# The first GEMM's leaky step on ScalarE's parametric rectifier, and attention's scales as a column

## The reference

```python
scores = q @ k.T / 8                       # 24 heads, 448 x 448, head_dim 64
scores = cap * tanh(scores / cap)          # cap = 30
x = softmax(scores) @ v                    # 896 x 768
h = x @ w_in                               # 768 x 2048: the first GEMM
g = maximum(0.01 * h, h)                   # the leaky step
x = g @ w_out                              # 2048 x 768: the second GEMM
xn = x / rms(x) * rms_g
out = (silu(xn @ w_gate) * (xn @ w_val)) @ w_out2   # 768 x 1536 twice, then 1536 x 768
```

## Time and profile before

| | us |
|---|---|
| median of 3 runs | 585.69 |
| lowest, highest | 584.68, 587.48 |
| the profiled execution | 586.64 |
| its span | 584.8 |
| PE busy | 571.6 (98%) |
| DVE busy | 386.7 (66%) |
| ACT busy | 261.2 (45%) |
| POOL busy | 273.2 (47%) |

### The profile page before, as it was taken

How to read it: one execution, slowest core, us unless ns; L and a number is a source line. 1 busy time by engine, 2 the same in 40 slices (tenths; PEclk the granted TensorE clock), 3 DMA queues, 4 the chain that set the end, 5 groups by cost and what they waited for, 6 DMA issues and landing times.

```text
span 584.8 us, 7734 instructions
## 1 busy us (share of the span) xinstructions
PE 571.6 (98%) x2805; PEld 491.1 (84%) x2805; DVE 386.7 (66%) x516; ACT 261.2 (45%) x428; POOL 273.2 (47%) x236
## 2 busy tenths in 40 slices
PE   5999999999999999999999999999999999999997
PEld 3555455599899999999999988999999999999997
DVE  4269798489978767334975498988888888511120
ACT  5787787414333344334643455443444434311110
POOL 1016455287855553333853477756687865100000
PEclk9999999999999999999999999999999999999999
DMA  6253442121311131111211011412111114100001
GB/s 166 78 184 110 126 122 62 34 72 55 108 55 54 55 109 59 55 53 28 78 54 54 0 56 54 163 59 92 67 54 55 55 54 139 52 27 28 28 27 55
DMA packets 30005, 41.48 MB, mean 71 GB/s; under 512 B 17040, under 2 KB 18960, under 8 KB 29968
## 3 DMA queue, kind: packets, MB, share of 16 engines
q1 hardware_dynamic: 29824, 40.99, 22.1%
q10 hardware_dynamic: 144, 0.00, 0.0%
HBM read 38.15 MB, written 2.80 MB: 70 GB/s over the span
## 4 chain that ended last, share of the span: by engine, by line
PE 87%; DVE 8%; issue 3%; DMA 1%; ACT 1%; DVEq 0%
PE ps L1325 38%; PE ps L1372 19%; PE ps L1449 15%; PE ps L1276 8%; PE ps L1257 3%; PE ps L1280 2%; PE ps L1261 1%; DVE s_sum L902 1%; DMA capc<-in_cap 1%; DVE x_lo L1080 1%; DVE g L955 1%; DVE s_sum L896 1%; DMA sums<-x_raw 1%; DVE x_raw L835 0%; DVE x_lo L1058 0%
## 5 line engine op out<-in xcount | busy, mean ns | idle before, releaser
L495 POOL TENSOR_TENSOR w_lo<-w_raw,w_hi 128x384 fp32r<-128x384 f32 x92 | 107.8, 1175 | 139.0 <-ACT w_hi L608 138.7
L1325 PE MATMUL ps<-x_hi,w_hi 128*128 128x448 f32 x420 | 154.5, 368 | 1.9 <-DVE a_t L918 1.1
L1325 PE MATMUL ps<-x_hi,w_lo 128*128 128x448 f32 x420 | 153.8, 366 | 0.0
L1325 PE MATMUL ps<-x_lo,w_hi 128*128 128x448 f32 x420 | 153.8, 366 | 0.0
L495 POOL TENSOR_TENSOR w_lo<-s_sum,w_hi 128x384 fp32r<-128x384 f32 x80 | 90.1, 1133 | 50.5 <-ACT w_hi L608 50.3
L1325 PEld LDWEIGHTS ps<-x_hi,w_hi 128*128 128x128 f32 x420 | 78.9, 188 | 10.6 <-issue 2.4
L1325 PEld LDWEIGHTS ps<-x_hi,w_lo 128*128 128x128 f32 x420 | 78.9, 188 | 6.9
L1325 PEld LDWEIGHTS ps<-x_lo,w_hi 128*128 128x128 f32 x420 | 78.9, 188 | 6.7
L608 ACT ACTIVATE w_hi<-s_sum 128x384 fp32r<-128x384 f32 x80 | 41.5, 523 | 81.2 <-PE ps L1325 67.7
L1276 PE MATMUL ps<-probs,v_ones 128*128 128x448 f32 x144 | 57.2, 547 | 0.9 <-DVE x_raw L835 0.8
L608 ACT ACTIVATE w_hi<-w_raw 128x384 fp32r<-128x384 f32 x92 | 47.2, 515 | 13.5 <-PE ps L1325 13.0
(11 more groups left out here) (141 smaller groups left out, 923.6 us busy)
## 6 DMA issues: line engine op xcount, KB each, us to landing
w_raw<-in_w_out SPq DMA_DIRECT2D x24, 384.0 KB, 3.1
w_raw<-in_w_in SPq DMA_DIRECT2D x16, 384.0 KB, 3.7
qk_raw<-in_qk SPq DMA_DIRECT2D x11, 480.0 KB, 4.2
w_raw<-in_w_gate SPq DMA_DIRECT2D x12, 384.0 KB, 3.0
w_raw<-in_w_val SPq DMA_DIRECT2D x12, 384.0 KB, 3.6
v_ones<-in_v SPq DMA_DIRECT2D x12, 224.0 KB, 3.2
recip_row<-recips SPq DMA_DIRECT2D x12, 224.0 KB, 3.3
v_raw<-in_w_out SPq DMA_DIRECT2D x4, 384.0 KB, 5.8
```

The source lines that it names most:

```text
L495: pool.tensor_tensor(w_lo[:, c], source, w_hi[:, c].bitcast(F32), ALU.subtract).then_inc(w_lo_done, 1)
L1325: last = pe.matmul(ps[:, base(s) + BANK_OF[j], 0:S], w[:, w_c], x[:, xs(j, c)], start=(j in (P1, P5, P7, P6) and c == 0 and w is w_hi and ...
```

## The change

The scales are read as columns of capc and no longer from registers. Block 11 is evicted from PSUM by ACT with Prelu and a slope of 0.01, in place of Copy; DVE's leaky step on it goes. For blocks 22, 12 and 21 the add stays on DVE, and a Prelu in place follows on ACT, behind a wait for c22_done, c12_done or c21_done. These are put between ACT's weight_hi steps: those of 22 and 12 of unit s stand near weight_hi(widx(s, 6) + 7), that of 21 behind keep_p1(s + 1), and for the last unit before g_hi(2). g_done counts three steps per unit, and g_hi waits for c11_kept besides.

```diff
@@ -583,12 +583,12 @@
                 act.wait_ge(scores_done, nth(p, i) + 1)
                 at_least(act, pv_done, p - 1)
                 act.activation(tiles(probs_of(p, i, n), S), ps[:, bank_of(p, i):bank_of(p, i) + n, 0:S],
-                               ACT.Tanh, scale=scale_reg).then_inc(tanh_done, 1)
+                               ACT.Tanh, scale=capc[:, 4:5]).then_inc(tanh_done, 1)
 
             def exp(p, half):
                 act.wait_ge(tanh_done, T * p + 2 * half + 2)
                 c = probs_of(p, 2 * half, 4 - half)
-                act.activation(c, c, ACT.Exp, scale=cap_reg, bias=capc[:, 6:7]).then_inc(exp_done, 1)
+                act.activation(c, c, ACT.Exp, scale=capc[:, 2:3], bias=capc[:, 6:7]).then_inc(exp_done, 1)
 
             def weight_hi(n):
 
@@ -613,15 +613,25 @@
                 at_least(act, u2_done, s - 1)
                 act.activation(p1[s % 2][:, :], ps[:, base(s) + BANK_A, 0:S], ACT.Copy).then_inc(p1_kept, 1)
 
-            def keep_11(s):
+            def hidden_11(s):
                 act.wait_ge(prod_done, count[widx(s, P2)])
-                act.activation(g_tile(4 * s), ps[:, base(s) + BANK_A, 0:S], ACT.Copy).then_inc(c11_kept, 1)
+                act.activation(g_tile(4 * s), ps[:, base(s) + BANK_A, 0:S], ACT.Prelu, alpha=0.01).then_inc(c11_kept, 1)
+
+
+            def leaky(s, b, taken):
+                act.wait_ge(taken, s + 1)
+                act.activation(g_tile(4 * s + b), g_tile(4 * s + b), ACT.Prelu, alpha=0.01).then_inc(g_done, 1)
+
+            def leaky_22_12(s):
+                leaky(s, 3, c22_done)
+                leaky(s, 1, c12_done)
 
             def g_hi(i):
 
                 f = i % N1
                 if i < N1:
-                    act.wait_ge(g_done, 4 * (f // 2 + 1))
+                    act.wait_ge(g_done, 3 * (f // 2 + 1))
+                    act.wait_ge(c11_kept, f // 2 + 1)
                 if i > 3:
                     act.wait_ge(prod_done, count[W_OUT + i - 4])
                 elif i > 1:
@@ -661,9 +671,6 @@
             act.wait_ge(qk_in[0], 16)
             act.activation(qk_hi[0][:, FIRST:QK], qk_raw[0][:, FIRST:QK], ACT.Copy).then_inc(qk_hi_done, 1)
             act.wait_ge(cap_done, 1)
-            cap_reg, scale_reg = act.alloc_register("cap_reg"), act.alloc_register("scale_reg")
-            act.reg_load(cap_reg, capc[0:1, 2:3].bitcast(mybir.dt.int32))
-            act.reg_load(scale_reg, capc[0:1, 4:5].bitcast(mybir.dt.int32))
 
             for p in range(PAIRS):
                 tanh(p, 0)
@@ -678,28 +685,30 @@
             for j in range(5):
                 weight_hi(widx(1, j))
             keep_p1(1)
-            keep_11(0)
+            hidden_11(0)
             weight_hi(widx(1, 5))
             weight_hi(widx(1, 6))
+            leaky_22_12(0)
             for j in range(5):
                 weight_hi(widx(2, j))
-            keep_11(1)
+            leaky(0, 2, c21_done)
+            hidden_11(1)
             weight_hi(widx(2, 5))
+            leaky_22_12(1)
             weight_hi(widx(2, 6))
             for s in range(2, U1):
                 keep_p1(s)
+                leaky(s - 1, 2, c21_done)
                 for j in range(5):
                     weight_hi(widx(s, j) + 7)
                 if s == U1 - 1:
                     g_hi(0)
                     g_hi(1)
-                keep_11(s)
-                if s < U1 - 1:
-                    weight_hi(widx(s + 1, 5))
-                    weight_hi(widx(s + 1, 6))
-
-            weight_hi(W_OUT + 5)
-            weight_hi(W_OUT + 6)
+                hidden_11(s)
+                weight_hi(widx(s, 5) + 7)
+                leaky_22_12(s)
+                weight_hi(widx(s, 6) + 7)
+            leaky(U1 - 1, 2, c21_done)
             g_hi(2)
             g_hi(3)
             for i in range(4, STEPS):
@@ -931,28 +940,15 @@
             def hidden_22(s):
                 dve.wait_ge(a2_done, s + 1)
                 dve.tensor_tensor(g_tile(4 * s + 3), bank(s, BANK_B), a_t[s % 2][:, :], ALU.add).then_inc(c22_done, 1)
-                dve.wait_ge(c22_done, s + 1)
-                leaky(4 * s + 3, g_tile(4 * s + 3))
 
             def hidden_12(s):
                 dve.wait_ge(u2_done, s + 1)
                 dve.wait_ge(prod_done, count[widx(s, P3)])
                 dve.tensor_tensor(g_tile(4 * s + 1), bank(s, BANK_C), u2[s % 2][:, :], ALU.add).then_inc(c12_done, 1)
-                dve.wait_ge(c12_done, s + 1)
-                leaky(4 * s + 1, g_tile(4 * s + 1))
-
-            def hidden_11(s):
-                dve.wait_ge(c11_kept, s + 1)
-                leaky(4 * s, g_tile(4 * s))
 
             def hidden_21(s):
                 dve.wait_ge(prod_done, count[widx(s, P4)])
                 dve.tensor_tensor(g_tile(4 * s + 2), bank(s, BANK_D), u2[s % 2][:, :], ALU.add).then_inc(c21_done, 1)
-                dve.wait_ge(c21_done, s + 1)
-                leaky(4 * s + 2, g_tile(4 * s + 2))
-
-            def leaky(k, h):
-                dve.scalar_tensor_tensor(h, h, 0.01, h, ALU.mult, ALU.max).then_inc(g_done, 1)
 
             def split_first():
                 c = slice(0, FIRST)
@@ -1007,9 +1003,7 @@
             take_p6(1)
             hidden_22(1)
             hidden_12(1)
-            hidden_11(0)
             hidden_21(0)
-            hidden_11(1)
             hidden_21(1)
             def g_lo(i):
                 f = i % N1
@@ -1037,7 +1031,6 @@
                 if s == U1 - 1:
                     g_lo(0)
                     g_lo(1)
-                hidden_11(s)
                 hidden_21(s)
 
             def out_bank(m, b):
```

## The result

| | before | changed |
|---|---|---|
| median of 20 runs, us | 585.17 | 583.99 |
| lowest, highest | 583.99, 589.3 | 583.2, 585.85 |
| the profiled execution | 586.64 | 584.55 |
| its span | 584.8 | 582.8 |
| ratio, 95% interval | | 0.9971 (0.9958 to 0.9985) |

The ratio is 1.7 us (0.9 to 2.5), the medians differ by 1.2, the two profiled executions by 2.1. The forecast stood on the median of three runs, 585.69; that of twenty is 585.17, so a part of what 584.9 is too high by lies in its starting point.

What follows compares the result with a forecast made beforehand. PE, busy 98% of the span, was taken to bound the kernel. The terms -1.11 - 0.1 + 0.2 + 0.2 = -0.8 us, from a median of 585.69, gave 584.9 us, range 582.7 to 587.7.

Steps and rivals of the forecast that it cites:

- What bounds: Whole kernel: PE is busy 98% of the span, so removing DVE work only moves the end where PE waits.
- The large stop: First GEMM, P3 of unit 2 at 147.80: PE's wait behind DVE's take_p5(2) goes, 1.11 us gained.
- The small stop: First GEMM, P4 of unit 1 at 137.31: PE's wait for POOL's w_lo(13) goes too, 0.1 us gained.
- rival A: First GEMM: small stop stays, large one goes, PE keeps 202.7 ns through 342 matmuls: 583.4 us; chance 0.17.
- "-0.1, +0.2": First GEMM: 0.1 us gained as the stop at 137.31 goes, 0.2 lost as 44 matmuls behind it stay slower.
- Pace: First GEMM: PE has two paces 4.0 ns per matmul apart, keeps one for hundreds of matmuls, changes at a stop.
- Prelu on ACT: First GEMM: Prelu takes 0.57 us each, 13.7 us for 24, and hides in ACT's idle time: cost 0.
- The rival of table switches: ACT: Prelu and Copy each load tables anew, up to six loads per unit: 8 us lost, 593; chance 0.02.
- Second GEMM: Start of the second GEMM: g_hi(2) comes 1.1 to 1.7 us later on ACT, nothing lost, at most 0.3.
- Columns: Attention: column scales cost 0.09 us per tanh and exp, hidden in the steady state; 0.2 us lost at the start.
- Rival B: Third stage: its 657 matmuls fall to 206.7 ns, 2.6 us lost, 587.5 in place of 584.9; chance 0.14.

Runs made afterwards that it cites:

- b1: The kernel before, unedited, run and profiled a second time: 587.2 us.
- b2: The kernel before, unedited, run and profiled a third time: 584.5 us.
- e3: The changed kernel with eight memsets (about 4 us of VectorE) in front of take_p5(2): ratio 1.0016 to the kernel before.
- e4: The kernel before with take_p5(2) moved in front of s_part(3) on DVE, all leaky steps still there: ratio 0.998.
- e1: The kernel before with only the scales of tanh and exp read as columns, leaky step still on DVE: ratio 1.0016.
- e8: The kernel before with take_p5(2) in front of s_part(3) and mean_square behind the first two s_parts of unit 10: 584.21 us, ratio 0.9971.
- e6: The changed kernel with P5 of unit 0 on PE waiting until P1 of unit 0 has ended: ratio 0.9976 to the kernel before.
- e7: The changed kernel with DVE's mean_square behind the first two s_parts of unit 10, not all four: ratio 0.9963 to the kernel before.
- a2: The changed kernel, unedited, run and profiled a third time: 584.1 us.
- a1: The changed kernel, unedited, run and profiled a second time: 583.3 us.

## Why the prediction was right, and where it was not

- *What bounds.* Right: PE's own rows gave the size. 29 us taken from DVE moved the end by under 2.
- *The large stop.* Right in place and in what came next. s_part(3) was held by its panel to 141.44 (worked out: 141.2), take_p5(2) came at 143.27. The 1.11 us was one execution's; in other executions the stop is 2.06, and the trace of one couldn't say so.
- *The small stop.* Wrong, and this is the step that failed. I argued that w_lo(13) would be quicker beside an idle DVE, and read the 2.37 us of the earlier trace rows as if both of the pair were slow. w_lo(13) had taken 1.01 us with DVE at work and took 1.02 without, so there was nothing to gain. It started 0.10 later, as everything did, and PE wants its weight load one matmul ahead, so the load was late by 0.23 as before. With the stop the quick pace behind it stayed too, and nothing threw it back: rival A, priced at 583.4, is what the profile shows. The terms "-0.1, +0.2" should have been 0 and -1.4 for the profiled pair. These 1.4 us are luck of the trace that I forecast from: two other executions of the kernel before (b1, b2) have the quick pace behind the large stop as well.
- *Pace.* That PE has two paces 4.0 ns apart held in every trace. e3 has the slower one without leaky steps on DVE, and e4 the quick one with all of them there, so it is not DVE's leaky work that sets it. Wrong is that I took the pace as the program's: behind the large stop it was the slower one in before, e1 and e3 and the quick one in b1 and b2. So a stop of 1 to 2 us was followed by a loss of 1.4 us more in three of five traces. Wrong as well is that it changes only at a stop: in e4 it changed behind a step that was 0.02 us too long, and in the second GEMM it changes without any, as the last section shows.
- *Prelu on ACT.* Right: 567 ns forecast as 570, no PE wait for ACT in this stage (the 0.2 us for probs are attention's). The eviction was free, 540 against 541. keep_p1(2) came at 141.83, worked out as 142.4. The rival of table switches was empty. The Trainium skill ("ScalarE: Activation LUTs", Rules for kernel authors) sends max and mul to VectorE; for this fp32 tile the runs differ from it, 567 ns on ACT against a mean of 1032 on DVE (624 to 1440 each).
- *Second GEMM.* Right. The changed kernel's g_lo(2) to (3) ran from 218.06 for 2.23 us, PE reached them at 223.35.
- *Columns.* The price per instruction was right (exp 1.79 to 1.88 us, tanh 0.92 to 1.01), and steady attention hid it: a pair takes 8.51 us in both. At the start 0.26 us was lost against 0.2 forecast. The kernel before has 7.10, 7.11 and 7.30 us for that stretch in its three traces, so the loss is 0.25 to 0.3 against two of them and under 0.1 against the third; why the third differs stays open.
- *Rival B.* The last 657 matmuls of the third stage kept 202.7 ns in all fourteen traces; some 40 ahead of them, up to 350 us, ran at either pace. Something else did come near there, which the forecast didn't have: the lower clock near 350 us. Its nine slow matmuls cost 1.5 us, and 0.57 in the end, since the wait for rms was then gone.

## What to carry to other kernels

When the bounding engine is busy for 98%, count its stops and read which single instruction ends each; moving 30 us of work off another engine was worth, in its stage, what moving one instruction ahead of its queue was worth (e4), and over the whole kernel no more than two such moves (e8). Compare the pace of equal instructions in different stretches before pricing a stop: the steps behind it can cost more than the stop. And take more than one profile of the kernel before, since one and the same stop had 1.1 us in one execution and 2.1 in the next.

## What the runs showed of the hardware

- In the first and the third stage, matmuls of 128 x 448 in fp32r run back to back at 202.7 or 206.7 ns at full granted clock. A pace lasted for up to 650 matmuls. Most changes came at a stop, even one in which only a weight load was late by 0.23 us; one (e4, 150.2) came behind a step of 0.23 us in place of 0.207. Behind the small stop at 137 us the pace was 202.7 ns in 11 of the 13 traces that have it (two of them, b1 and e6, had it before), and 206.7 in e4 and e7. What distinguishes the two was not found.
- In the second GEMM the same matmuls change their mean pace every 36, with no step over 0.21 us. These are the first three groups of 36 in the kernel before, 205.3, 202.5 and 205.3 ns each:

```profile
218.56:225.95 7.39, 7.39 (x38) 6.76 (x37) 6.57 (x10) 3.37 (x8) 2.42 (x2) 1.00 0.17 55
225.95:233.24 7.29, 7.29 (x38) 6.76 (x37) 4.48 (x6) 3.29 (x8) 3.26 (x3) 1.00 0.17 54
233.24:240.63 7.39, 7.39 (x37) 6.75 (x36) 2.32 (x4) 2.92 (x6) 2.22 (x2) 1.00 0.17 53
```

  In all fourteen traces the odd groups have 205.3 ns or so (204.4 in the seventh and the fifteenth) and most of the even ones 202.5 to 203; the tenth has 206.6 in each.
- The granted clock fell to its lower level for 3 to 4 us behind pauses of about 2 us, in some executions only: behind the pause at 348 to 350 us in the first profile of the changed kernel and in a2, and not in a1; behind the large stop in e1 and e3, not in b1. From start to start of the matmuls around it the pause was 2.2 us at 348 us in all three, 2.4 and 2.2 us in e1 and e3, and 2.4 in b1. The slow matmuls, 0.37 us each, cost some 1.5 us each time. Behind the stops of 1.1 us (1.5 from start to start) it did not fall.
